# Where z and x are split and how x is transposed: a linear-attention, mixing and gated network on one core

## The reference, cut to what matters

```
# attention: f = sigmoid(f_logit)
state = f[t][:, None] * state + k[t] outer v[t];  y[t] = q[t] @ state
# x = y, (4, 768, 384); mixing
u  = x + (relu(x.T @ w_tok1) @ w_tok2).T          # 768 -> 256 -> 768, over tokens
z  = u + relu(u @ w_ch1) @ w_ch2                  # 384 -> 1536 -> 384
# gated
h  = relu(z @ w_in)                               # 384 -> 1024
c  = conv_w[0]*h[s-1] + conv_w[1]*h[s] + conv_w[2]*h[s+1]
out = (h * sigmoid(c)) @ w_out                    # 1024 -> 384
```

## Time and profile before

| | us |
|---|---|
| median of 3 runs (755.74 to 757.6) | 757.33 |
| profiled execution | 755.4 |
| its span, first to last instruction | 753.7 |
| PE busy | 687.5 |
| DVE busy | 427.1 |
| ACT busy | 208.4 |
| POOL busy | 132.1 |

### The profile page before, as it was taken

One profiled execution on the slowest core, in us unless ns is written; L12 is line 12 of the kernel. 1 busy time (PEld: TensorE's weight loads), 2 busy tenths in 40 slices (PEclk: granted clock), 3 DMA queues, 4 the chain that ended last, 5 costly groups with the idle time before them and its releaser, 6 DMA issues.

```text
span 753.7 us, 13556 instructions
## 1 busy us (share of the span) xinstructions
PE 687.5 (91%) x5192; PEld 663.1 (88%) x5192; DVE 427.1 (57%) x722; ACT 208.4 (28%) x382; POOL 132.1 (18%) x100
## 2 busy tenths in 40 slices
PE   2674999999999999899999999989898998998997
PEld 1664999999999999899999999989897997997996
DVE  5896155673355583345575321333777777777774
ACT  1332122221122211122221122111443443444442
POOL 3536021120012110011211025620003003003000
PEclk9955899999999999999999999999999999999999
DMA  6576012210411210222120022200200300300101
GB/s 181 161 193 136 2 33 67 61 44 1 113 36 44 83 45 1 65 65 64 44 85 30 3 80 80 75 31 1 94 1 0 127 1 0 125 0 0 63 0 63
DMA packets 45964, 43.31 MB, mean 57 GB/s; under 512 B 3824, under 2 KB 42992, under 8 KB 45904
## 3 DMA queue, kind: packets, MB, share of 16 engines
q1 hardware_dynamic: 44992, 39.34, 17.9%
q0 software_dynamic: 912, 3.16, 1.4%
HBM read 33.04 MB, written 9.44 MB: 56 GB/s over the span
## 4 chain that ended last, share of the span: by engine, by line
PE 74%; DVE 15%; issue 4%; ACT 3%; DMA 2%; POOL 1%; DVEq 0%; SPq 0%; ACTq 0%; POOLq 0%
PE bank L421 66%; DVE conv_acc L985 3%; PE bank L448 3%; PE bank L470 2%; DVE p_sb L795 2%; DVE conv_acc L982 1%; PE bank L477 1%; DVE z_out L943 1%; DVE g_l L969 1%; PE bank L437 1%; PE bank L459 1%; DMA stage<-in_moe_w_ch 1%; DVE attn L821 1%; ACT g_h L763 1%; DVE z_out L939 1%
## 5 line engine op out<-in xcount | busy, mean ns | idle before, releaser
L922 DVE SCALAR_TENSOR_TENSOR h_l<-bank,h_h 128x384 fp32r<-128x384 f32 x96 | 53.0, 555 | 153.8 <-ACT h_h L709 153.8
L709 ACT ACTIVATE h_h<-bank 128x384 fp32r<-128x384 f32 x96 | 47.2, 491 | 256.6 <-PE bank L421 256.6
L421 PE MATMUL bank<-h_h,w_ch_h 128*128 128x384 f32 x288 | 101.1, 351 | 3.1 <-DVE h_l L922 2.8
L421 PE MATMUL bank<-h_h,w_ch_l 128*128 128x384 f32 x288 | 96.5, 335 | 0.0
L421 PE MATMUL bank<-u_h,w_ch_l 128*128 128x384 f32 x288 | 96.4, 335 | 0.0
L421 PE MATMUL bank<-h_l,w_ch_h 128*128 128x384 f32 x288 | 96.4, 335 | 0.0
L421 PE MATMUL bank<-u_h,w_ch_h 128*128 128x384 f32 x288 | 96.2, 334 | 0.0
L421 PE MATMUL bank<-u_l,w_ch_h 128*128 128x384 f32 x288 | 96.2, 334 | 0.0
L363 POOL TENSOR_TENSOR k_sc<-k_raw,inv_p 128x512 f32<-128x512 f32 x24 | 30.7, 1280 | 312.1 <-DVE inv_p L802 312.1
L421 PE MATMUL bank<-w_out_h,g_h 128*128 128x384 f32 x192 | 66.3, 345 | 13.4 <-DVE g_l L969 13.4
L985 DVE SCALAR_TENSOR_TENSOR conv_acc<-h_sb,conv_sb,conv_acc 128x768 f32<-128x768 f32 x64 | 73.9, 1154 | 2.3
(11 more groups left out here) (112 smaller groups left out, 1268.5 us busy)
## 6 DMA issues: line engine op xcount, KB each, us to landing
f_raw<-in_f_t SPq DMA_DIRECT2D x48, 96.0 KB, 2.6
k_raw<-in_k_t SPq DMA_DIRECT2D x48, 96.0 KB, 2.6
q_raw<-in_q_t SPq DMA_DIRECT2D x48, 96.0 KB, 2.6
v_nat<-in_v_rows SPq DMA_DIRECT2D x24, 192.0 KB, 2.8
stage<-in_moe_w_ch SPq DMA_DIRECT2D x6, 768.0 KB, 4.6
z_scratch<-z_out SPq DMA_DIRECT2D x24, 192.0 KB, 2.1
z_in<-z_scratch SPq DMA_DIRECT2D x4, 1152.0 KB, 5.3
out<-y_out SPq DMA_DIRECT2D x24, 192.0 KB, 1.9
```

The costliest lines, as they stand in the source:

```text
L421: mm = pe.matmul(dst, stationary(a), moving(c), start=start and n == 0, stop=stop and n == len(parts_) - 1, **kw)
L709: act.activation(h2_hl[0][n % 2][:, :], mix[3 + n % 2][:, 0:HALF], ACT.Relu).then_inc(h2_hi, 1)
L922: dve.scalar_tensor_tensor(h2_hl[1][n % 2][:, :], mix[3 + n % 2][:, 0:HALF], 0.0, h2_hl[0][n % 2][:, :].bitcast(F32), ALU.max, ALU.subtrac ...
```

## The change

It moves the split of z from the gated stage to the mixing stage: `top_of_z` on ACT and `low_of_z` on POOL write the two parts, which are stored apart and loaded straight into the operand tiles, with two such pairs of tiles. ACT keeps y in fp32 as `x_full` and rounds from there; POOL makes the low part of x (`low_of_x`). PE transposes `x_full` with the transposing mode of the matmul. k is scaled in place, `causal` is one block broadcast four times, and the gated loops are written out. Cut to its core, with the indentation less by eight. New semaphores, and the same edits in the path that takes the attention step by step when decays are very small, are left out:

```diff
-    z_dram = nc.dram_tensor("z_scratch", (B, DM, S), F32).ap()
+    z_dram = [nc.dram_tensor(f"z_scratch_{x}", (B, DM, S), F32).ap() for x in "hl"]
...
 z_out = sb("z_out", [P, KD, HALF], F32, mixing)
+z_top = stage[0][:, 0:KD * HALF].rearrange("p (k s) -> p k s", k=KD).bitcast(F32R)
+z_low = z_out[:, :, :].bitcast(F32R)
...
 x_hl = [sb(f"x_{x}", [P, NCH, DM], F32R, early) for x in "hl"]
+x_full = sb("x_full", [P, NCH, DM], F32, early)
...
 v_nat = [sb(f"v_nat{i}", [P, DM], F32, early) for i in range(2)]
-causal = sb("causal", [P, NPR, P], F32, early)
+causal = sb("causal", [P, 1, P], F32, early)
...
 ident = sb("ident", [P, P], F32, early)
-ident_r = sb("ident_r", [P, P], F32R, early)
...
 w_out_hl = [sb(f"w_out_{x}", [P, FF, DM], F32R) for x in "hl"]
-z_hl = [sb(f"z_{x}", [P, KD, S], F32R) for x in "hl"]
-z_in = sb("z_in", [P, KD, S])
+z_hl = [[sb(f"z_{x}{i}", [P, KD, S], F32R) for x in "hl"] for i in range(2)]
...
         at = slice(c * P, (c + 1) * P)
-        for x, tile, here, used in ((f_t, f_raw, f_here, decays), (k_t, k_raw, k_here, k_scaled),
+        for x, tile, here, used in ((f_t, f_raw, f_here, decays), (k_t, k_raw, k_here, scores),
...
         for d in range(KD):
-            wait(sp, z_done, NU * b + KD * half + d + 1)
+            at = z_dram[0][b, d * P:(d + 1) * P, half * HALF:(half + 1) * HALF]
+            wait(sp, z_high, NU * b + KD * half + d + 1)
             sp.sem_inc(passed, 1)
-            sp.dma_start(z_dram[b, d * P:(d + 1) * P, half * HALF:(half + 1) * HALF],
-                         z_out[:, d, :]).then_inc(z_kept[d], 16)
+            sp.dma_start(at, z_top[:, d, :].bitcast(F32)).then_inc(z_kept[d], 16)
+        for d in range(KD):
+            at = z_dram[1][b, d * P:(d + 1) * P, half * HALF:(half + 1) * HALF]
+            wait(sp, z_lows, NU * b + KD * half + d + 1)
+            sp.sem_inc(passed, 1)
+            sp.dma_start(at, z_low[:, d, :].bitcast(F32)).then_inc(z_kept[d], 16)
...
         for d in range(KD):
-            wait(sp, z_kept[d], 32 * (b + 1))
-        wait(sp, z_split_lo, KD * b)
+            wait(sp, z_kept[d], 64 * (b + 1))
+        wait(sp, in_ps, 2 * FF * (b - 1))
         sp.sem_inc(passed, 1)
-        sp.dma_start(z_in[:, :, :], z_dram[b, :, :].rearrange("(k p) s -> p k s", p=P)).then_inc(z_here, 16)
+        for to, src in zip(z_hl[b % 2], z_dram):
+            sp.dma_start(to[:, :, :].bitcast(F32),
+                         src[b, :, :].rearrange("(k p) s -> p k s", p=P)).then_inc(z_here[b % 2], 16)
...
     z_load(0)
+    z_load(1)
...
     z_store(B - 1, 1)
-    with sp.Fori(0, B - 1) as b:
-        z_load(b + 1)
+    for b in range(B):
+        if b + 2 < B:
+            z_load(b + 2)
         y_store(b)
-    y_store(B - 1)
...
-    pool.affine_select(out=causal[:, :, :], in_=causal[:, :, :], compare_op=ALU.is_ge, fill=0.0,
-                       base=0, pattern=[[0, NPR], [1, P]], channel_multiplier=-1).then_inc(consts, 1)
+    pool.affine_select(out=causal[:, 0, :], in_=causal[:, 0, :], compare_op=ALU.is_ge, fill=0.0,
+                       base=0, pattern=[[1, P]], channel_multiplier=-1).then_inc(consts, 1)
...
         here = 32 * (NCH // 2 * b + c // 2 + 1)
-        wait(pool, scores, g)
+        k = k_raw[c % 2][:, :, :]
...
         wait(pool, inverses, g + 1)
-        pool.tensor_tensor(k_sc[:, :, :], k_raw[c % 2][:, :, :], inv_p[:, :, :], ALU.mult).then_inc(k_scaled, 1)
+        pool.tensor_tensor(k, k, inv_p[:, :, :], ALU.mult).then_inc(k_scaled, 1)
...
     pool.wait_ge(pads, 6)
-    pool.wait_ge(consts, 9)
-    pool.tensor_copy(ident_r[:, :], ident[:, :]).then_inc(consts, 1)
+
+    def low_of_x(b, c):
+        g = NCH * b + c
+        wait(pool, x_hi, g + 1)
+        pool.tensor_tensor(x_hl[1][:, c, :], x_full[:, c, :], x_hl[0][:, c, :].bitcast(F32),
+                           ALU.subtract).then_inc(x_lo, 1)
...
         scale(0, c)
+        if c > 1:
+            low_of_x(0, c - 2)
...
         odd_low(n)
+    low_of_x(0, NCH - 2)
+    low_of_x(0, NCH - 1)
...
                        allow_slow_non_contiguous=True).then_inc(conv_here, 16)
+    def low_of_z(b, half):
+        for d in range(KD):
+            wait(pool, z_high, NU * b + KD * half + d + 1)
+            pool.tensor_tensor(z_low[:, d, :], z_out[:, d, :], z_top[:, d, :].bitcast(F32),
+                               ALU.subtract).then_inc(z_lows, 1)
+
...
             scale(b, c)
+            if c > 1:
+                low_of_x(b, c - 2)
+            if c == NCH - 2:
+                low_of_z(b - 1, 0)
+        low_of_x(b, NCH - 2)
+        low_of_x(b, NCH - 1)
+        low_of_z(b - 1, 1)
...
-    def split_z(b):
-
-        for kt in range(KD):
-            wait(pool, z_split_hi, KD * b + kt + 1)
-            pool.tensor_tensor(z_hl[1][:, kt, :], z_in[:, kt, :], z_hl[0][:, kt, :].bitcast(F32),
-                               ALU.subtract).then_inc(z_split_lo, 1)
-
...
             load(n + 1)
-    split_z(0)
-    with pool.Fori(1, B) as b:
-        split_z(b)
+        if i == 2:
+            low_of_z(B - 1, 0)
+    low_of_z(B - 1, 1)
...
                 for p in range(NPR):
-                    mm = pe.transpose(kt_bank(b)[:, p * P:(p + 1) * P], k_sc[:, p, :], ident[:, :])
+                    mm = pe.transpose(kt_bank(b)[:, p * P:(p + 1) * P], k_raw[c % 2][:, p, :], ident[:, :])
...
             else:
-                wait(pe, x_lo, g)
+                wait(pe, x_kept, g)
...
                     rows = slice(h * HP, h * HP + D)
-                    mm = pe.matmul(dst[:, p * P:(p + 1) * P], k_sc[rows, p, :], q_sc[c % 2][rows, p, :],
+                    mm = pe.matmul(dst[:, p * P:(p + 1) * P], k_raw[c % 2][rows, p, :], q_sc[c % 2][rows, p, :],
...
             for c in range(HCH):
-                product(dst[:, c * P:(c + 1) * P],
-                        lambda a: x_hl[a][:, half * HCH + c, d * P:(d + 1) * P],
-                        lambda a: ident_r[:, :], c == 0, False, ((0, 0), (1, 0)), skip_group_check=True)
+                pe.matmul(dst[:, c * P:(c + 1) * P], x_full[:, half * HCH + c, d * P:(d + 1) * P],
+                          ident[:, :], start=c == 0, stop=False, is_transpose=True, skip_group_check=True)
...
         for half in range(2):
-            if f == 0:
-                if isinstance(b, int) and b == 0:
+            if f == 0 and half == 0:
+                wait(pe, z_here[b % 2], 32 * (b // 2 + 1))
+                if b == 0:
...
             for kt in range(KD):
-                if f == 0:
-                    wait(pe, z_split_lo, KD * b + kt + 1)
                 mm = product(bank[3 + half][:, 0:HALF], lambda a: w_in_hl[a][:, kt, f * P:(f + 1) * P],
-                             lambda a: z_hl[a][:, kt, half * HALF:(half + 1) * HALF], kt == 0, kt == KD - 1)
+                             lambda a: z_hl[b % 2][a][:, kt, half * HALF:(half + 1) * HALF],
+                             kt == 0, kt == KD - 1)
...
             if f == 0:
-                if isinstance(b, int) and b == 0:
+                if b == 0:
                     wait(pe, z_part, NU * B)
-                    wait(pe, x_lo, NCH * B)
+                    wait(pe, x_kept, NCH * B)
...
             wait(act, y_done, g + 1)
-            act.activation(x_hl[0][:, c, :], y_bank(b, c)[:, 0:DM], ACT.Copy,
-                           accum_out=y_sum[:, c:c + 1]).then_inc(x_hi, 1)
+            act.activation(x_full[:, c, :], y_bank(b, c)[:, 0:DM], ACT.Copy,
+                           accum_out=y_sum[:, c:c + 1]).then_inc(x_kept, 1)
+            wait(act, x_kept, g + 1)
+            act.activation(x_hl[0][:, c, :], x_full[:, c, :], ACT.Copy).then_inc(x_hi, 1)
...
-    def split_z(b):
-        wait(act, in_ps, 2 * FF * b)
-        wait(act, z_here, 16 * (b + 1))
-        for kt in range(KD):
-            act.activation(z_hl[0][:, kt, :], z_in[:, kt, :], ACT.Copy).then_inc(z_split_hi, 1)
+    def top_of_z(b, half):
+        for d in range(KD):
+            wait(act, z_done, NU * b + KD * half + d + 1)
+            act.activation(z_top[:, d, :], z_out[:, d, :], ACT.Copy).then_inc(z_high, 1)
...
                     slot(nxt, *stage_)
-            elif n == FC // 2:
-                split_z(0)
+            if n == FC + 2:
+                top_of_z(b, 0)
...
             settle(nxt)
+        top_of_z(b, 1)
...
                 gated_hi(b, f - 1)
-            if f == FF - 1 and nxt is not None:
-                split_z(nxt)
...
             act.activation(gate[f % 2][:, :], conv_acc[f % 2][:, :], ACT.Sigmoid).then_inc(gates, 1)
-            if f == 0 and not (isinstance(b, int) and b == 0):
+            if f == 0 and b:
...
                 dve.tensor_tensor(attn[h][:, :, :], src[:, :].rearrange("p (a t) -> p a t", a=NPR),
-                                  causal[:, :, :], ALU.mult).then_inc(masked, 1)
+                                  causal[:, :, :].to_broadcast([P, NPR, P]), ALU.mult).then_inc(masked, 1)
...
                 ins.then_inc(states, 1)
-            wait(dve, x_hi, g + 1)
```

(32 more changed lines are left out.)

6 lines of the change are left out of this document (2 added, 4 removed).

## The result

The changed kernel took 736.48 us (median of 4 runs, 735.13 to 736.68); the kernel before, in the same rounds, 757.44 (755.74 to 757.6). The ratio is 0.9724 [0.9706, 0.9743], so 21.0 us less. The forecast was 740.5 and its range 734.5 to 748. The profiled execution took 736.35, its span 734.5, against 755.4 and 753.7. Those are four executions each. Run again beside each other, with more executions of the kernel before, they took 756.21 and 735.91 (e0_after), 20.3 us apart. One of the later executions of the kernel before took 1959.7 us, in the slow state, and no comparison uses it.

The account below looks back on a forecast made before the run. TensorE, busy 91% of the span, was taken to bound the kernel, idling mainly in the opening and at hand-overs. Terms summed to -16.05 on 755.4: 739.4, or 741.3 by the median; forecast 740.5, range 734.5 to 748.

Parts of the forecast that it names:

- The hand-overs: Between batches' gated stages: without POOL's z split TensorE's idle goes, -10.7, plus -1.6 for a clock fall behind the third.
- the two waits: First hand-over: TensorE waits 1.35 for z's low part and 2.30 for the delayed gated product; both go.
- the slack of the product: First hand-over: gated product ready at 577.7, TensorE asks at 578.6, so nothing is late next, by 0.9 us.
- The last mixing stage: POOL's weight piece and z split no longer hold DVE's z additions, so TensorE's 2.25 idle before 494.01 goes: -2.25.
- The start of the gated stage: POOL's z subtractions meet DVE's first convolution step, one instruction of delay: +0.95, bounds 0 and 2.9; 2.5 us idle.
- The transposes: Token groups: three fp32 transposing matmuls replace six, 0.11 each, gain 0.24 in 20 groups: -4.8, bounds -6.7 and +2.6.
- The rival of a falling clock: Rival 4: clock falls where x is transposed, in the four token sections: 747, or 781 if long; chance 0.03.
- The opening: First batch's attention: POOL's low parts of x delay weights and the v load: +2.35, bounds -1 and +5.
- The 0.35 and 0.85: Opening: first weight pair 0.35 late from ACT's second copy; DVE's scans 0.85 late from chunk 1's low part.
- The mixing stages: Mixing stages 0 to 2: added ACT copies, POOL subtractions and SP stores cost nothing: 0.
- Rival 3: POOL's subtractions hold DVE in the mixing stages; if each costs TensorE 0.96, +40: 781; chance 0.03.
- the first of the signs of being wrong: DVE rows held beside POOL rows in the mixing stages would show the prediction wrong.

Follow-up runs that it names:

- e0_after: The changed kernel again without any edit, as the anchor for the follow-up runs: 735.91 us, ratio 0.9739 to the kernel before.
- pool_again: Changed kernel plus three POOL subtractions of 768 columns on spare memory at each of three hand-overs, nothing waiting for them: 756.59 us, ratio 1.0006.
- x_only: Kernel before plus the x half of the change (x_full, low part on POOL, transposing mode, k scaled in place), z split as before: 752.94 us.
- unroll: Kernel before with only the loops of the gated stages written out: 757.08 us, ratio 1.0007.
- pair_T: Changed kernel with x transposed as before, six fp32r matmuls with an identity per group: 741.89 us, ratio 0.9812.
- turn_first: Changed kernel with the transposes of a batch's first three groups issued before the first token product: 733.96 us, ratio 0.9711.
- xlow_dve: Changed kernel with the low part of x made by DVE out of PSUM instead of by POOL: 734.19 us, ratio 0.9718.
- v_early: Changed kernel, opening: last v chunk loaded before the last weight piece, POOL's last low parts of x before its last weight subtraction: 736.31 us.
- all_dve: Changed kernel with turn_first, first tile's product parts earlier in batches 1 to 3, early v load on SP alone, low part of x on DVE: 728.59 us.
- all_three: Changed kernel with turn_first, v_early and the first tile's product parts made earlier in batches 1 to 3: 732.10 us, ratio 0.9693.

## Why the prediction was right, step by step

**The hand-overs** (-10.7, measured -13.7 with the clock). The mechanism is shown by pool_again. It also shows that the two waits were not independent: without the wait for z the product would have been waited for 3.98 in one piece, so by this run taking away that wait alone would have given nothing. The sum came out because the change took away both. Three sizes were off. First, an idle piece costs more than its length: in the old hand-over the start-to-start distance over the 1.35 piece was 1.68, where 0.17 is the pace, and the next matmul came after 0.28 instead of 0.17, so 1.62 in all; 0.27 on top of each of six pieces is 1.6 of the gain. Second, the slack of the product is 0.43, not 0.9; with nothing late it changed no sum. Third, the clock: -1.6 was assumed, and the third stage gained 1.2 to 1.35 more than the other two. In all three profiles with the old hand-overs the clock fell behind one of them (the third in before and x_only, the second in unroll); of the eleven others it fell there in pool_again alone.

**The last mixing stage** (-2.25, -2.5): as argued, plus the same 0.27.

**The start of the gated stage** (+0.95, +0.7): the idle piece went from 1.58 to 1.99, not to 2.5. DVE was held by the rest of POOL's last subtraction, not by all of it: its second and third step took 2.70 instead of 2.07.

**The transposes** (-4.8, -5.9, and 6.0 by pair_T). The 0.11 each was right; the way out was taken as 0.11 to 0.20 from the attention's burst, and is 0.03 into a token product: 205.03 to 205.44 is 0.42, and with the next two matmuls a group gains 0.34. The first group of a batch did gain nothing, as forecast: its idle time grew by what it saved (0.56 to 0.84). Five groups make 1.7, which is what the second and the fourth token section gained; the first gained 1.2, since more of it now ran at half clock, and the third 1.3, having lost 0.5 ahead of its first token product. The rival of a falling clock gets no support: from 82.3 us on the clock was 1.0 through the token sections of this execution, the half clock before that came over from the opening, and where another execution had a fall in a token section it came ahead of the first transpose (turn_first).

**The opening** (+2.35, +1.43 in this pair). The v load moved by 1.1 (63.59 to 64.68), which is the one low part of 1.11 in front of it. The 0.35 and 0.85 that I had followed through from earlier chunks did not reach it here. At the first pair DVE began first, 39.81 against POOL's 39.94, and had its own 1.76; the wait moved to its next step (3.40 on four columns). That order is not the change's doing: in e0_after, the same kernel, POOL began first (39.54 against 39.83) and DVE's subtraction took 4.88. DVE is free again within 0.9 of the old time either way (44.07 before, 44.88 and 44.71 in the two). In the six other profiles of this order the v load came at 64.86 to 65.59. The last leg, from TensorE's restart to the first mixing matmul, grew by 0.55, not 0.15. xlow_dve gives the total back. How far the 0.35 and 0.85 reach in those later openings was not followed.

**The mixing stages** (0, measured +0.9). This term was put at nothing and was not: Rival 3 exists in a small form, and the first of the signs of being wrong came true. At one attention step of each stage POOL's low part of x stands beside DVE's update of the state:

```profile
272.06 2.19 DVE L859 TENSOR_TENSOR state<-state,carry 48x192 f32<-48x192 f32 x2
...
272.90 1.13 POOL L383 TENSOR_TENSOR x_l<-x_full,x_h 128x384 fp32r<-128x384 f32 x1
```

Before, without POOL's row, it took 1.45:

```profile
273.49 1.45 DVE L841 TENSOR_TENSOR state<-state,carry 48x192 f32<-48x192 f32 x2
```

The next chunk's four transposes on TensorE wait for this state update, and 0.19 to 0.21 is lost there in each of the three stages. In the first a wait of 0.19 ahead of 155.71 went in exchange, so 0.5 is left in all. The other 0.4 is an idle piece at the mixing loop's end, 1.97 before and 2.37 here, which was 1.96 in e0_after, the same kernel. xlow_dve did not return the 0.5 (99.55 in its first mixing stage against 99.25 in e0_after), and its rows say why: there POOL's low part of z stands beside the same update, which takes 2.18. x_only, which splits no z in these stages, has it at 2.17 beside the low part of x. So a POOL subtraction beside the update goes with the cost in each of these traces; a kernel with none beside it was run only as the one before.

**Open.** Why the clock falls behind some idle pieces and not others. Behind 3.98 us it fell each time. Behind about 2 us, at the mixing loop's end and at the start of the gated stages, it fell in some executions (turn_first, v_early, all_dve; at the second place also all_three) and not in the others. The old hand-overs, 3.5 us in two pieces, drew it at one of three. Each such step in a token section cost 1.6 us, so differences of that size between single executions mean little. The profiled run of before, 755.4, is no riddle: the 42 other executions of the kernel before that count took 753.88 to 758.73; it was the median of the first four, 757.44, that lay high.

## What to carry to other kernels

Price a GpSimd instruction that reads SBUF by the VectorE instructions standing beside it and by who waits for those: one of one column on the chain costs as much as a long one, and an instruction nobody waits for can take back a whole change. Look for a place where VectorE reads PSUM or idles, or leave the work to VectorE where it can take it from PSUM: the low part of h, a VectorE step with one of its inputs in PSUM, took 0.56 at 393.21 with POOL's subtractions running beside it, and 0.56 in the kernel before without them. Count TensorE's idle pieces with what follows them, 0.27 us each here and a step of half clock behind the one of 3.98; shorter pieces are worth removing even where the busy share is already 92%. And compare more than one profile before a difference of 1 to 2 us in a stage is put down to an edit: the opening moved by 1.3 between profiles of one order.

## What the runs showed of the hardware that was not expected

The cost of POOL's load at the hand-over isn't proportional: 4.1 us for one subtraction in each of three places, 20.7 for three. After 3.98 us without a matmul the granted clock stood at 0.50 for 6.83 us, three times out of three; after 1.06, three places, it stayed at 1.0. A 128x1 operation of DVE took 2.88 us beside POOL's, a 128x4 copy 3.40. Three fp32 blocks of 128 x 128 in transposing mode cost TensorE 0.42 us, from the start of the matmul ahead to the start of the one behind, with the clock at 1.0 throughout.
